# Pooled attention: row maxima in eleven pieces instead of fifteen, seven of them before the first values

## What is computed

```
q_pool = q.reshape(B, H, S // 2, 2, D).mean(axis=3)          # S = 1152, D = 64
scores = D ** -0.5 * np.matmul(q_pool, k.transpose(0, 1, 3, 2))
scores = scores - np.max(scores, axis=-1, keepdims=True)
attn = np.exp(scores)
attn = attn / (np.sum(attn, axis=-1, keepdims=True) + 1e-09)
out = np.matmul(attn, v)
```

## Time and profile before

| | |
|---|---|
| median of three runs | 1186.14 us |
| the profiled execution, its own time | 1188.16 us |
| its span | 1186.4 us |
| busy in the span: PE, weight loads (PEld) | 1122.6 us, 930.4 us |
| busy: DVE, ACT, POOL | 806.3 us, 620.1 us, 675.0 us |
| first and last start of a piece's reduction (L647) | 22.7 us, 506.5 us |
| L382, 465 matmuls of pieces | 165.9 us in all, mean 379 ns |
| L647, 465 reductions | 250.4 us in all, mean 556 ns |

### The profile page before, as it was taken

One profiled execution on the slowest core, in us unless ns is written; L12 is line 12 of the kernel. 1 busy time (PEld: TensorE's weight loads), 2 busy tenths in 40 slices (PEclk: granted clock), 3 DMA queues, 4 the chain that ended last, 5 costly groups with the idle time before them and its releaser, 6 DMA issues. The chain is left out here.

```text
span 1186.4 us, 19899 instructions
## 1 busy us (share of the span) xinstructions
PE 1122.6 (95%) x7088; PEld 930.4 (78%) x7088; DVE 806.3 (68%) x1573; ACT 620.1 (52%) x1228; POOL 675.0 (57%) x689
## 2 busy tenths in 40 slices
PE   6999999989999999998898989879999999999998
PEld 4777777777878777787777777558888888888887
DVE  5788877767888888866556565665548754686554
ACT  4666665566666666656565656543334333443331
POOL 5888899998888888734233335522344333533330
PEclk9999999999999999998999999999999999999999
DMA  8211112211122221001001002122222512223121
GB/s 206 61 57 53 48 56 61 60 42 51 61 61 61 60 61 41 22 1 36 1 1 38 5 29 67 58 93 96 65 72 58 173 58 68 71 60 118 55 71 54
DMA packets 76593, 71.47 MB, mean 60 GB/s; under 512 B 11856, under 2 KB 54864, under 8 KB 76496
## 3 DMA queue, kind: packets, MB, share of 16 engines
q1 hardware_dynamic: 75888, 69.90, 19.7%
q10 hardware_dynamic: 608, 0.30, 0.1%
HBM read 60.74 MB, written 9.44 MB: 59 GB/s over the span
## 5 line engine op out<-in xcount | busy, mean ns | idle before, releaser
L647 DVE TENSOR_REDUCE part_max<-psA 128x1 f32<-128x384 f32 x465 | 250.4, 556 | 59.4 <-PE psA L382 37.3
L576 ACT ACTIVATE pT<-psA 128x576 f32<-128x576 f32 x288 | 187.7, 652 | 165.5 <-PE psA L401 156.6
L270 POOL TENSOR_TENSOR pT<-pT 128x576 f32<-128x576 f32 x157 | 225.6, 1437 | 26.3 <-ACT pT L576 4.3
L2155 DVE TENSOR_TENSOR hidden_parts<-psC,hidden_parts 128x384 f32<-128x384 f32 x168 | 90.8, 553 | 129.3 <-PE psC L2003 120.1
L382 PE MATMUL psA<-kT,qT 128*128 128x384 f32 x465 | 165.9, 379 | 11.4 <-DVE part_max L647 11.0
L415 PE MATMUL psA<-pT,v_raw 128*64 128x288 f32 x1152 | 153.9, 412 | 0.0
L1828 POOL TENSOR_TENSOR w_raw<-w_raw 128x256 f32<-128x256 f32 x24 | 18.3, 763 | 217.9 <-DMA w_raw<-in_moe_w_ch 217.7
L392 PE MATMUL psA<-qT,kT 128*128 128x288 f32 x576 | 132.3, 311 | 0.0
L401 PE MATMUL psA<-qTm,kT 128*128 128x288 f32 x576 | 123.1, 295 | 0.5 <-ACT qTm L562 0.5
L415 PEld LDWEIGHTS psA<-pT,v_raw 128*64 128x64 f32 x1152 | 77.0, 137 | 53.2 <-issue 6.4
L392 PEld LDWEIGHTS psA<-qT,kT 128*128 128x128 f32 x576 | 98.4, 189 | 18.4 <-issue 14.0
(11 more groups left out here) (197 smaller groups left out, 2616.7 us busy)
## 6 DMA issues: line engine op xcount, KB each, us to landing
w_raw<-in_moe_w_ch SPq DMA_DIRECT2D x48, 256.0 KB, 3.1
k_raw<-in_k SPq DMA_DIRECT2D x32, 288.0 KB, 2.9
v_raw<-in_v SPq DMA_DIRECT2D x32, 288.0 KB, 2.8
q_raw<-in_q SPq DMA_DIRECT2D x31, 256.0 KB, 3.3
w_even<-in_moe_w_ch SPq DMA_DIRECT2D x12, 512.0 KB, 5.0
w_odd<-in_moe_w_ch SPq DMA_DIRECT2D x12, 512.0 KB, 5.0
u_rows<-x_all SPq DMA_DIRECT2D x16, 256.0 KB, 2.0
u_even<-u_rows SPq DMA_DIRECT2D x2, 1536.0 KB, 6.7
```

Source lines behind the costliest of these rows:

```text
L270: nc.gpsimd.tensor_tensor(pT[:, KT, :], pT[:, KT, :], pT[:, j, :], ALU.add).then_inc(part_summed, 1)
L576: nc.scalar.activation(pT[:, j, :].rearrange("p (a c) -> p a c", a=2), scores[n % 2][:, :, 0:HALF], ACT.Exp, scale=0.5 * float(D) ** -0.5) ...
L647: nc.vector.tensor_reduce(part_max[u][:, t, c:c + 1], maxes[n % 2][:, 0:PIECE], AX.X, ALU.max).then_inc(max_freed[n % 2], 1)
L2155: nc.vector.tensor_tensor(to, session((k, n))[:, 0:W], other, ALU.add).then_inc(added, 1)
```

## The change

The first pass is cut otherwise. Row tiles 0 to 3 take keys 0 to 511 in one matmul of 512 columns each ("a"), keys 512 to 1023 in another ("b"), and the last 128 keys of all four tiles together in one bank, four matmuls of 128 columns, with one reduction that writes four maxima ("c"). The last row tile, with its 64 queries, is laid twice in `qT`, once in rows 0 to 63 and once shifted by 64, so that two matmuls summed in one bank give the first half of the keys on partitions 0 to 63 and the second half on 64 to 127 ("half", 512 columns and then 64). That makes eleven pieces. `maximum` first joins the two partition halves by a small reduction (64 x 2 to 64 x 1), waits for it, and then reduces four entries a tile instead of three. ACT's copy of the last query tile writes 256 columns instead of 128. On PE, seven pieces (0 to 6) stand in front of the early values, `turn_out` and `sum_rows` stand side by side just in front of those values, and the last piece between scores 6 and 7. In the list of the last head `turn_out`, `sum_rows` and `normalise` move behind two transposes of x.

```diff
-    PIECES = ([(t, c) for c in range(2) for t in range(QT - 1)] + [(QT - 1, 0), (QT - 1, 1)]
-              + [(t, 2) for t in range(QT)])
+    PIECES = ([("a", t) for t in range(QT - 1)] + [("b", t) for t in range(QT - 1)]
+              + [("c", None), ("half", 0), ("half", 1)])
+    HALF_KEYS = S // 2
@@ max_piece on PE
-                nc.tensor.matmul(maxes[n % 2][:, 0:PIECE], qT[h % 3][:, t * P:(t + 1) * P],
-                                 kT[u][:, c * PIECE:(c + 1) * PIECE], start=True, stop=True
-                                 ).then_inc(max_filled, 1)
+                if kind == "half":
+                    a, z = ((0, BANK), (BANK, HALF_KEYS))[t]
+
+                    parts = [(out[:, 0:z - a], q[:, c:c + P],
+                              k[:, m * HALF_KEYS + a:m * HALF_KEYS + z])
+                             for m, c in enumerate(((QT - 1) * P, SQ))]
+                elif kind == "c":
+                    parts = [(out[:, t * P:(t + 1) * P], q[:, t * P:(t + 1) * P], k[:, 2 * BANK:S])
+                             for t in range(QT - 1)]
+                else:
+                    at = 0 if kind == "a" else BANK
+                    parts = [(out, q[:, t * P:(t + 1) * P], k[:, at:at + BANK])]
+                for m, (to, queries, keys) in enumerate(parts):
+                    mm = nc.tensor.matmul(to, queries, keys, start=kind != "half" or m == 0,
+                                          stop=kind != "half" or m == 1)
+                mm.then_inc(max_filled, 1)
@@ copy_keys on ACT
-                    nc.scalar.activation(qT[h % 3][:, 4 * P:WIDE], turn[:, P:2 * P], ACT.Copy)
+                    nc.scalar.activation(
+                        qT[h % 3][:, 4 * P:].rearrange("p (n c) -> p n c", c=P),
+                        turn[:, P:2 * P].unsqueeze(1).to_broadcast([P, 2, P]), ACT.Copy)
@@ maximum on DVE
-                    dve.wait_ge(max_freed[n % 2], n // 2 + 1)
+                    for m in (n - 1, n):
+                        dve.wait_ge(max_freed[m % 2], m // 2 + 1)
+
+                    nc.vector.tensor_reduce(part_max[u][0:LAST, QT - 1, 2:3],
+                                            part_max[u][LAST:P, QT - 1, 0:2], AX.X, ALU.max
+                                            ).then_inc(halves_moved, 1)
+                    dve.wait_ge(halves_moved, h)
@@ the loop on PE
+                score(h, 3)
                 maxima(4, 5)
-                score(h, 3)
-                maxima(5, 6)
+                score(h, 4)
+                maxima(5, 7)
+
                 if h > 0:
                     turn_out(h - 1)
-                maxima(6, 7)
-                if h > 0:
                     sum_rows(h - 1)
-                maxima(7, 8)
-                score(h, 4)
-                maxima(8, 9)
                 values(h, range(EARLY))
-                maxima(9, 11)
+                maxima(7, 9)
                 score(h, 5)
-                maxima(11, 12)
+                maxima(9, 10)
                 if more2:
                     turn_keys(h + 2, "ka", range(0, 4))
-                maxima(12, 13)
                 score(h, 6)
-                maxima(13, 14)
+                maxima(10, 11)
                 score(h, 7)
-                maxima(14, 15)
                 score(h, 8)
```

More of the change, by code:

```diff
@@ L30 @@
 MASKED = -1000000000.0
+LOWEST = -3.0e38
 def ceil_div(a, b):
@@ L120, in attention @@
         kT1 = [sb(f"kT1{u}", [P, S], F32R) for u in range(2)]
-        qT = [sb(f"qT{u}", [P, WIDE], F32R) for u in range(3)]
+        qT = [sb(f"qT{u}", [P, WIDE + P], F32R) for u in range(3)]
         qTm = [sb(f"qTm{u}", [P, WIDE], F32R) for u in range(2)]
-        part_max = [sb(f"part_max{u}", [P, QT, 3]) for u in range(2)]
+        part_max = [sb(f"part_max{u}", [P, QT, 4]) for u in range(2)]
         pT = sb("pT", [P, KT + 1, SQ])
@@ L154, in attention @@
         wide_reduced = sem("wide_maxima_reduced")
+        halves_moved = sem("halves_moved")
         padded = sem("padding_written")
@@ L182, in attention @@
         block = ctx.enter_context(nc.Block())
-        PADS = 8
+        PADS = 10
         def load_q(eng, h):
@@ L372, in max_piece @@
             def max_piece(h, at):
-                u, (t, c) = h % 2, PIECES[at]
+                u, (kind, t) = h % 2, PIECES[at]
                 n = max_no(h, at)
+                out, q, k = maxes[n % 2], qT[h % 3], kT[u]
                 if at == 0:
                     pe.wait_ge(qa_copied, h + 1)
-                for first, name in (((0, 0), "ka"), ((0, 1), "kb"), ((QT - 1, 0), "kc")):
-                    if (t, c) == first:
+                for first, name in ((("a", 0), "ka"), (("b", 0), "kb"), (("c", None), "kc")):
+                    if PIECES[at] == first:
                         pe.wait_ge(turn_freed, keys_before[name, h] + 1)
@@ L499, in _ @@
             first(0, ("x", 2))
-            turn_out(h - 1)
-            sum_rows(h - 1)
             first(0, ("x", 3))
@@ L504, in _ @@
             first(0, ("x_last",))
+            turn_out(h - 1)
+            sum_rows(h - 1)
             values(h, range(EARLY))
@@ L644, in max_piece @@
             def max_piece(h, at):
-                u, (t, c), n = h % 2, PIECES[at], max_no(h, at)
+                u, (kind, t), n = h % 2, PIECES[at], max_no(h, at)
+                src = maxes[n % 2]
                 dve.wait_ge(max_filled, n + 1)
-                nc.vector.tensor_reduce(part_max[u][:, t, c:c + 1], maxes[n % 2][:, 0:PIECE],
-                                        AX.X, ALU.max).then_inc(max_freed[n % 2], 1)
+                if kind == "half":
+                    to = part_max[u][:, QT - 1, t:t + 1]
+                    src = src[:, 0:BANK if t == 0 else HALF_KEYS - BANK]
+                elif kind == "c":
+                    to = part_max[u][:, 0:QT - 1, 2]
+                    src = src.rearrange("p (t k) -> p t k", k=P)
+                else:
+                    c = 0 if kind == "a" else 1
+                    to = part_max[u][:, t, c:c + 1]
+                nc.vector.tensor_reduce(to, src, AX.X, ALU.max).then_inc(max_freed[n % 2], 1)
             def wide_maxima(t):
                 dve.wait_ge(wide_filled, t + 1)
-                nc.vector.tensor_reduce(part_max[0][:, t, :], wide(t), AX.X, ALU.max
+                nc.vector.tensor_reduce(part_max[0][:, t, 0:3], wide(t), AX.X, ALU.max
                                         ).then_inc(wide_reduced, 1)
@@ L716, in _ @@
             nc.vector.memset(oT[:, HALF + SHIFT:3 * P], 0.0).then_inc(padded, 1)
+            nc.vector.memset(part_max[0][:, :, 3:4], LOWEST).then_inc(padded, 1)
+            nc.vector.memset(part_max[1][:, :, 2:4], LOWEST).then_inc(padded, 1)
             nc.vector.memset(group_sums[:, SQ // BLOCK:], 0.0).then_inc(padded, 1)
@@ L736, in _ @@
                 for at in range(len(PIECES)):
-                    if at == 9 and h > 0:
+                    if at == 7 and h > 0:
                         normalise(h - 1)
@@ L760, in _ @@
             first(0, ("x", 2))
-            normalise(h - 1)
             first(0, ("x", 3))
             first(0, ("x_last",))
+            normalise(h - 1)
             add_tile(5, 0)
```

## The result

The changed kernel took 1194.9 us, the median of five runs (1194.11 to 1196.6), against 1186.23 (1184.57 to 1188.42, five runs): a ratio of 1.008 with a 95% interval of 1.0066 to 1.0094, so it is slower by 7.8 to 11.2 us. The prediction said 1192.0 within 1183 to 1196, and slower with a chance of 0.65.

The account below looks back on a forecast made before the run. Steady heads were held bound by PE with two chains (piece, reduction, same bank; score 6, exponent 6, score 8), seven heads by POOL. 22 to 23 turns x 0.27 gave 6 us over the 1186.14 median: 1192, range 1183 to 1196.

Parts of the forecast that it names:

- Two regimes: Whole head loop: 21 steady heads paced by PE and chains get longer; 7 middle heads follow POOL and change by 0.
- PE's work: First pass: 2.96 us instead of 2.6, 0.3 us more a head, with short matmuls at 0.11 us each.
- The chain of a bank: Two pieces in one bank start at least 1.28 us apart instead of 1.09; 1.17 up to the weight load.
- The way through the head: Steady head, start by start: lateness passes from early values to score 6, score 8 and the tail; 0.27 us a head.
- Early values: Steady head: early values start 8.4 us after the late ones, 8.3 before; net 0.1 us late.
- Score 6: Steady head, behind piece 9 and the turned key tiles: 0.4 us late, the sum of 0.1, 0.19 and 0.11.
- Score 8: Steady head: hangs on exponent 6 and is late by the same 0.4 us as score 6.
- The wait for exponent 6: PE ahead of score 8: about 0.28 us of waiting instead of 0.14.
- The transposes of `q_lo_m`: Tail of a steady head: 0.1 us of waiting goes, since the last piece is now early.
- the last head's list: The move in the last head: concerns one head, 0.3 us at most either way.
- It gets faster: Rival: PE's stops on DVE go and none replace them; some 10 us less, 1176, or half, 1181; chance 0.15.
- No change: Rival: lateness shrinks to about 0.1 us a steady head; 1188 to 1189 us; chance 0.2.

Follow-up runs that it names:

- e5: The changed kernel with the four short matmuls of piece 8 replaced by one of 512 columns; 1193.65 us, ratio 1.0056 to the kernel before.
- e6: e3 with the four short matmuls of piece 8 replaced by one of 512 columns; 1178.4 us, ratio 0.9927 to the kernel before.
- e10: The changed kernel without the reduction joining the two partition halves and without its wait; 1192.57 us, ratio 1.0064 to the kernel before.
- e3: The changed kernel with piece 6 between `turn_out` and `sum_rows`, piece 8 behind score 5, piece 9 behind score 6; 1180.4 us, ratio 0.9948.
- e8: e3 with piece 1 behind the turned last key tile, piece 2 behind score 2, piece 3 behind the turned queries; 1177.3 us, ratio 0.9918.
- e9: e8 with `turn_out`, `sum_rows` and `normalise` in the last head placed as before the change; 1175.93 us, ratio 0.9917.

## Why the prediction was right, point by point

The direction, the place of the loss and the chain behind it were as forecast, and the time lies in the range, 2.9 us over the point. The size of the sum was less good, and some of its agreement is luck, as told below.

*Two regimes.* Right. The 21 steady heads carry the change, 2.54 us in the first stretch and 4.09 in the last; the seven POOL heads lost nothing, and even gave 1.05 us back. A PE that is slower before them may leave POOL less to catch up; that was not tested.

*PE's work.* Four matmuls of 128 columns at the price of their weights: the row from 414.60 has five matmuls, and score 5 starts 0.73 us behind the first (415.33). If the first takes its 0.33, 0.10 is left for each of the four. I had 0.11. I also had them off the path, hidden by the chain from piece 7 to piece 9, and that was wrong by a hair: with them PE's own work from piece 7 to piece 9 is 1.32 us, the chain 1.28. e5 shows that taking them out gains nothing by itself.

*The chain of a bank.* 1.17 us up to the next weight load was measured as 1.18 at piece 6; 1.28 from start to start was measured as 1.28 in e5. At piece 6 the matmuls lose 0.30 us (0.76 from piece 5 to `turn_out`, less two of 0.23), forecast 0.29; the 0.35 in brackets is the idle time of the weight load. The wait of 0.1 us that I expected for the load of piece 9 is not in the list of waits; its trace is the 0.53 us from piece 9 to the turned keys instead of 0.46.

*The way through the head*, each counted from the late values. Early values: 8.44 us in the changed kernel (412.51 less 404.07), 8.3 before; forecast 8.4. Score 6: 12.67, against 12.32; forecast 0.4 later, measured 0.35. Score 8: 0.41 later (14.17 against 13.76), forecast 0.4. The wait for exponent 6: 0.23, forecast 0.28. The transposes of `q_lo_m` no longer wait: 0.93 us behind score 8 (418.24 to 419.17) instead of 1.03, the 0.1 of the forecast.

*The sum.* This is where it was off. The steps added up to 0.3 us, and I wrote "with the roundings all upward, I take 0.27"; they were not, it was 0.31, and 21 heads make 6.6 us instead of 5.7. By the rows a head is 0.35 late at score 6 (forecast 0.4), gathers 0.06 more up to score 8 (1.50 us between the two for 1.44 before), where I had nothing, and gets 0.10 back in the tail. The 0.35 hide two misses that go against each other: 1.32 us instead of 1.28 from piece 7 to piece 9, and 0.82 instead of 0.93 from piece 9 to score 6, because piece 9 was not stopped for long and its restart cost less. The other small term, the last head's list, I had bounded at 0.3 us "either way"; it cost 0.6, since I did not look at which bank the fourth tile of x needs. Against it stand 1.05 us from the middle and 1.06 from the ends. Of these, 0.62 are the last full turn, 14.54 us from 497.86 where it was 15.16 from 492.72; I had counted it as 0.27 longer. The other 0.44 come from the first two turns, of which the second was unusually long in the trace before. In the trace the late values of the last full head therefore come 4.5 us later (512.40, before 507.88), and the span is 6.3 us longer. That the terms I had wrong or had at nothing nearly cancel is luck.

*What stays open.* The medians differ by 8.7 us, the profiled executions by 6.3. The profiled execution before was itself 1.9 us over its median (1188.16). What follows on attention, whose code no kernel here changes behind the last head, took between 674.8 and 680.3 us in the traces looked at, among them 678.5 before and 680.3 after. The granted clock goes with a part of it: it was 0.991 over the span before and 0.987 after, and 0.99 against 0.98 from those late values to the end. A difference of 0.004 over 1190 us is at most 4.8 us, an estimate. Of the twelve traces only e6's shows 0.98 there as well, and those two stretches are the longest, 680.3 and 679.6 us. And e5 and e10, whose steady heads are as long as the changed kernel's, came out 6.3 and 7.4 us over the kernel before on their chips, so the 8.7 may itself be 1 or 2 us high. A single trace cannot assign the last 2 us.

*The rivals.* "It gets faster" was priced on the waits of the old order, and its condition, pieces ready more than 1.28 us apart by themselves, is what e3 and e8 make true by hand: there it came out, at 1177 us in e8, close to the 1176 that the rival had. In the changed kernel itself half of the condition held: pieces 7 and 9 are 1.32 us apart by PE's work alone, where I had found 1.2, and pieces 4 and 6 would be 1.00 apart (410.43 to 411.20 and one width of 0.23), where I had 0.99. "No change" failed by its size.

## What to carry to other kernels

With two banks taking turns between a producer and a consumer, what counts is the time from the start of a piece to the start of the next piece in the same bank: fill, consume, signal, load. Widening the pieces makes that chain longer even when it makes the consumer's total shorter, so wide pieces need more other work between neighbours; count for each pair of pieces of one bank what lies between them. Where the work in between is as long as the chain, as from piece 7 to piece 9, shortening one of the two gains next to nothing. A matmul engine that shows 99.9% busy can still lose 0.3 us in 15 at such places, and start times show it where busy time does not.

## What the runs showed that I had not expected

The same eleven pieces, in an order that keeps them apart, beat both kernels: 1175.93 us in e9, 9 us under the kernel before on that chip, although PE does more work in each head. And in the order of e6 one engine's saving came out at half, because every second head waits for DVE; I had taken a steady loop to have one length.
